# Agent attention with a gated feed-forward layer on one core: value pairs with a shared column of ones, a reciprocal column, and a new order of loads

## The reference

```python
# q, k, v: (2, 12480, 128); agents: (2, 49, 128); w_in (128, 2048), w_out (2048, 128), alpha (2048)
def sm(a, b):
    s = scale * (a @ b.transpose(0, 2, 1))
    s = s - s.max(-1, keepdims=True)
    e = np.exp(s)
    return e / (e.sum(-1, keepdims=True) + 1e-09)
agent_v = sm(agents, k) @ v
x = (sm(q, agents) @ agent_v).reshape(24960, 128)
h = x @ w_in
g = np.maximum(h, 0.0) + alpha * np.minimum(h, 0.0)
out = g @ w_out
```

## Time and profile before

| | us |
|---|---|
| median of three runs | 929.99 |
| the profiled execution | 929.73 |
| its span (first to last instruction) | 928.0 |
| PE busy | 911.3 |
| DVE busy | 627.2 |
| ACT busy | 515.1 |
| POOL busy | 108.4 |

### The profile page before, as it was taken

One profiled execution on the slowest core, in us unless ns is written; L12 is line 12 of the kernel. 1 busy time (PEld: TensorE's weight loads), 2 busy tenths in 40 slices (PEclk: granted clock), 3 DMA queues, 4 the chain that ended last, 5 costly groups with the idle time before them and its releaser, 6 DMA issues.

```text
span 928.0 us, 16051 instructions
## 1 busy us (share of the span) xinstructions
PE 911.3 (98%) x5642; PEld 488.6 (53%) x5642; DVE 627.2 (68%) x914; ACT 515.1 (56%) x695; POOL 108.4 (12%) x138
## 2 busy tenths in 40 slices
PE   8898999999999999999999999999999999999998
PEld 8874555555546556654545444444444444444443
DVE  4555666676777767767767676666767676767664
ACT  2344555556565555555556565656555555555654
POOL 5310100101001001001001010101010101010101
PEclk9998999999999999999999999999999999999999
DMA  8951222322222322211111111111111111111110
GB/s 302 301 162 50 81 77 60 101 57 67 82 71 92 99 71 89 68 36 59 35 38 54 36 59 35 58 34 54 39 52 41 49 43 45 48 40 52 41 33 22
DMA packets 74149, 65.75 MB, mean 71 GB/s; under 512 B 38528, under 2 KB 69760, under 8 KB 73856
## 3 DMA queue, kind: packets, MB, share of 16 engines
q1 hardware_dynamic: 73824, 65.19, 23.3%
q10 hardware_dynamic: 288, 0.06, 0.0%
HBM read 40.49 MB, written 12.78 MB: 57 GB/s over the span
## 4 chain that ended last, share of the span: by engine, by line
PE 93%; DMA 3%; SPq 2%; issue 2%; DVE 0%; POOLq 0%; ACT 0%
PE ps L574 55%; PE ps L557 18%; PE ps L564 7%; PE ps L538 3%; PE ps L584 2%; DMA kv_s<-kT 2%; PE ps L736 2%; PE ps L418 2%; PE ps L730 1%; PE ps L496 1%; SPq L288 1%; DMA q_s<-qT 1%; DMA PT<-stack 1%; PE ps L519 1%; PE ps L449 0%
## 5 line engine op out<-in xcount | busy, mean ns | idle before, releaser
L1142 DVE SCALAR_TENSOR_TENSOR r_lo<-ps,r_hi 128x960 f16<-128x960 f32 x416 | 466.6, 1153 | 250.8 <-ACT r_hi L897 248.4
L897 ACT ACTIVATE r_hi<-ps 128x960 f16<-128x960 f32 x416 | 386.2, 967 | 175.8 <-PE ps L564 175.7
L574 PE MATMUL ps<-r_hi,w_hi 128*128 128x480 f16 x832 | 252.4, 369 | 4.0 <-DMA q_s<-qT 3.7
L574 PE MATMUL ps<-r_hi,w_lo 128*128 128x480 f16 x832 | 248.4, 367 | 0.0
L574 PE MATMUL ps<-r_lo,w_hi 128*128 128x480 f16 x832 | 241.1, 367 | 0.0
L557 PE MATMUL ps<-PT,M_a 128*128 128x480 f16 x832 | 204.0, 367 | 0.2 <-DVE r_lo L1142 0.2
L403 POOL TENSOR_TENSOR y<-y_relu,y_lin 128x480 f32<-128x480 f32 x52 | 62.4, 1200 | 622.2 <-ACT y_relu L980 449.8
L574 PEld LDWEIGHTS ps<-r_hi,w_lo 128*128 128x128 f16 x832 | 91.4, 111 | 68.8
L557 PEld LDWEIGHTS ps<-PT,M_a 128*128 128x128 f16 x832 | 81.3, 99 | 86.8 <-DVE r_lo L1142 2.0
L574 PEld LDWEIGHTS ps<-r_lo,w_hi 128*128 128x128 f16 x832 | 85.6, 106 | 71.2
L574 PEld LDWEIGHTS ps<-r_hi,w_hi 128*128 128x128 f16 x832 | 73.0, 106 | 87.5 <-issue 43.4
(11 more groups left out here) (147 smaller groups left out, 526.1 us busy)
## 6 DMA issues: line engine op xcount, KB each, us to landing
q_s<-qT SPq DMA_DIRECT2D x52, 240.0 KB, 2.6
out<-y SPq DMA_DIRECT2D x52, 240.0 KB, 2.0
kv_s<-kT SPq DMA_DIRECT2D x24, 512.0 KB, 4.3
kv_s<-vP SPq DMA_DIRECT2D x12, 512.0 KB, 7.1
kv_s<-vS SPq DMA_DIRECT2D x8, 768.0 KB, 4.4
PR<-PT SPq DMA_DIRECT2D x156, 32.0 KB, 1.8
PT<-stack SPq DMA_TRANSPOSE x208, 2.4
w_lin<-w_out SPq DMA_DIRECT2D x1, 1024.0 KB, 8.4
```

What stands on the lines that cost most here:

```text
L574: mm = pe.matmul(ps[:, OUT, 0:CHUNK], w[:, 2 * p + u, :], r[:, s, u, :], start=(p == 0 and u == 0 and k == 0), stop=(p == PAIRS - 1 and u ...
L897: act.activation(r_hi[:, p % RING, :, :], ps[:, at:at + 2, 0:CHUNK], ACT.Relu).then_inc(hi_ready, 1)
L1142: dve.scalar_tensor_tensor(out=r_lo[:, p % RING, :, :], in0=ps[:, at:at + 2, 0:CHUNK], scalar=0.0, in1=r_hi[:, p % RING, :, :], op0=ALU.ma ...
```

## The change

Five things are changed; the diff is cut to them.

1. w_inT is loaded after the last key piece, and relu_max_row is worked after piece 11 instead of 10.
2. Tiles of values lie in pairs: a column of ones, two tiles of 128 channels, and the next pair's column of ones behind (RUN = 257). An even tile is multiplied with the ones ahead of it, an odd one with the ones behind. A load writes runs of 256 floats. The ones are written slot by slot.
3. ACT and DVE first copy the column of sums alone (den_col); PE multiplies it by `pairs` (two identity halves side by side, so that both halves' sums are added and stand on the rows of both), DVE adds EPS and takes the reciprocal of one column, scales sel by it, and turn_values multiplies by that matrix. PE's order around it and the places of the eight key tiles change.
4. SP: chunk 3 is loaded ahead of the bodies, and body n loads chunk n + 4 into its own place after q_scored(n + 3). `turn` is split: turn(0, 0), the transposes, stands ahead of k_tail and key piece (1, 0), and `spread(0, 0)`, the copies, behind them.
5. The mixes of batch 0 use other banks, the first body starts its second layer on r_low and lo_ready(1), runs second_layer(0) without key tiles, starts the second group after m_low(3), and works the key tiles in second_layer(1) and second_layer(2).

```diff
@@ -20,6 +20,7 @@
 VC = C + 1
+RUN = 2 * C + 1
 TAIL = (N - FULL * PIECE) // 2
@@ -79,9 +80,9 @@
-        kv_s = sb("kv_s", [128, 2 * RING, 8 * VC])
+        kv_s = sb("kv_s", [128, 2 * RING, 4 * RUN + 1])
         k_tail = sb("k_tail", [C, B, 2 * TAIL])
-        v_tail = sb("v_tail", [TAIL, B, 2, VC])
+        v_tail = sb("v_tail", [TAIL, B, RUN + 1])
         S = sb("S", [KT, B, TILES, A])
@@ -90,9 +91,12 @@
         rec = sb("rec", [C, A])
-        rec_sel = sb("rec_sel", [C, SEL])
-        av_rows = sb("av_rows", [128, VC])
-        den_sel = sb("den_sel", [128, SEL])
...
+        av_rows = sb("av_rows", [128, VC + 1])
+        pairs = sb("pairs", [128, 128])
+        den_col = sb("den_col", [128, 1])
+        rec_col = sb("rec_col", [128, 1])
+        rec_sel = sb("rec_sel", [128, SEL])
         av_acc = sb("av_acc", [C, A])
@@ -136,7 +140,7 @@
         W_BANK, K_BANK = 4, 5
-        F_BANK = (4, OUT, 4, 5)
+        F_BANK = (4, 4, 5, SMALL)
         REST_BANK, LIN_BANK = (OUT, SMALL), (5, SMALL)
@@ -223,12 +227,14 @@
-        def values_in(m):
-            return kv_s[:, value_slot(m), :].rearrange("p (t c) -> p t c", c=VC)
...
-        def ones_of(s):
-            return kv_s[:, s:s + RING, :].rearrange("p s (t c) -> p (s t) c", c=VC)[:, :, C:VC]
...
+        def with_ones(t):
+            at = t // 2 * RUN + t % 2 * VC
+            return slice(at, at + VC)
...
+        def without_ones(x):
+            return x.rearrange("p (j c) -> p j c", c=RUN)[:, :, 1:RUN]
@@ -248,27 +254,28 @@
                     sp.wait_ge(v_used, m - 2 * RING + 1)
-                sp.dma_start(values_in(m)[:, :, 0:C], vP[m - 1].rearrange("p (t c) -> p t c", c=C)).then_inc(in_v[(m - 1) % (2 * RING)], 16)
+                sp.dma_start(without_ones(kv_s[:, value_slot(m), 0:4 * RUN]),
+                             vP[m - 1].rearrange("p (j c) -> p j c", c=2 * C)).then_inc(in_v[(m - 1) % (2 * RING)], 16)
             def load_tail(b):
-                sp.dma_start(v_tail[:, b, :, 0:C], vTail[b].rearrange("p (t c) -> p t c", c=C)).then_inc(in_vt[b], 16)
+                sp.dma_start(v_tail[:, b, 1:RUN], vTail[b]).then_inc(in_vt[b], 16)
...
                     sp.dma_start(w_lin[:, :, :], w_out).then_inc(in_wo, 16)
-                if m == FULL - 2:
-                    sp.dma_start(w_inT_s[:, :, :], w_inT).then_inc(in_wT, 16)
+            sp.dma_start(w_inT_s[:, :, :], w_inT).then_inc(in_wT, 16)
             sp.dma_start(q_s[:, 0, :], qT[0]).then_inc(in_q[0], 16)
...
                 load_values(m)
...
-            sp.wait_ge(q_scored, 1)
-            sp.dma_start(q_s[:, 0, :], qT[2]).then_inc(in_q[0], 16)
+            for n in range(2):
...
+                sp.wait_ge(q_scored, n + 1)
+                sp.dma_start(q_s[:, n, :], qT[n + 2]).then_inc(in_q[n], 16)
@@ -287,27 +294,31 @@
+            def spread(n, half):
...
                 sp.wait_ge(q_turned, 64 * n + 64)
...
+            turn(0, 0)
...
             sp.dma_start(kv_s[:, 2, 0:PIECE], kT[1, 0]).then_inc(in_k[2], 16)
-            turn(0, 0)
+            spread(0, 0)
             for h in range(2):
...
             turn(1, 1)
+            spread(1, 1)
...
                     n = 2 * i + half
-                    if there(n + 3):
...
-                        sp.wait_ge(q_scored, n + 2)
-                        sp.dma_start(q_s[:, 1 - half, :], qT[n + 3]).then_inc(in_q[1 - half], 16)
+                    if there(n + 4):
...
+                        sp.wait_ge(q_scored, n + 3)
+                        sp.dma_start(q_s[:, half, :], qT[n + 4]).then_inc(in_q[half], 16)
                     if kind == KEYS and (not isinstance(n, int) or n + 2 + EARLY <= FULL):
@@ -324,6 +335,7 @@
                         turn(n + 2, half, n)
+                        spread(n + 2, half)
@@ -484,27 +496,29 @@
-                pe.wait_ge(ones_in, 2 if m <= RING else 3)
+                pe.wait_ge(ones_in, RING + 1 if m <= RING else 2 * RING + 1)
                 pe.wait_ge(k_exped, m + 1)
...
                     if m == 0:
-                        rhs, rows = v_tail[:, 0, t, :], TAIL
+                        rhs, rows = v_tail[:, 0, with_ones(t)], TAIL
                     else:
-                        rhs, rows = values_in(m)[:, t, :], KT
+                        rhs, rows = kv_s[:, value_slot(m), with_ones(t)], KT
...
+            def denominators_paired():
+                pe.wait_ge(b_dencol, 2)
+                pe.matmul(ps[:, K_BANK, 0:1], pairs[:, :], den_col[:, :], start=True, stop=True).then_inc(b_den, 1)
...
             def turn_values():
                 pe.wait_ge(b_rows, 2)
-                pe.matmul(ps[:, W_BANK, 0:SEL], av_rows[:, 0:C], sel[:, :], start=True, stop=True).then_inc(b_turned, 1)
...
-            def denominators_spread():
-                pe.wait_ge(b_spread, 2)
-                pe.matmul(ps[:, K_BANK, 0:SEL], ones[:, :], den_sel[:, :], start=True, stop=True).then_inc(b_den, 1)
+                pe.wait_ge(b_recsel, 1)
+                pe.matmul(ps[:, W_BANK, 0:SEL], av_rows[:, 1:VC], rec_sel[:, :], start=True, stop=True).then_inc(b_turned, 1)
@@ -590,7 +604,7 @@
                 first_scores(m)
-                if m == FULL - 2:
+                if m == FULL - 1:
@@ -636,21 +650,22 @@
+            pe.wait_ge(b_shift, 1)
+            denominators_paired()
+            pe.wait_ge(in_k[2], 16 * (FULL // RING + 1))
+            piece_scores(2, 2, range(0, 3))
...
             pe.wait_ge(wmax_ready, 1)
             turn_values()
...
-            pe.wait_ge(b_shift, 1)
-            denominators_spread()
-            pe.wait_ge(in_k[2], 16 * (FULL // RING + 1))
-            piece_scores(2, 2, range(0, 4))
+            piece_scores(2, 2, range(3, 5))
...
             value_sums(0, K_BANK)
+            piece_scores(2, 2, range(5, 8))
...
             query_scores(0)
-            piece_scores(2, 2, range(4, 8))
@@ -666,8 +681,10 @@
             mix(0, 1, F_BANK[1])
+            pe.wait_ge(l_low, 1)
             mix(0, 2, F_BANK[2])
-            pe.wait_ge(l_low, 1)
...
+            pe.wait_ge(q_shifted, 3)
             mix(0, 3, F_BANK[3])
@@ -690,7 +707,7 @@
-                        pe.wait_ge(m_low, 2)
+                        pe.wait_ge(r_low, 1)
                         pe.wait_ge(lo_ready, 1)
@@ -699,7 +716,7 @@
-                    if kind != PLAIN and not (kind == MIX_REST and half == 1):
+                    if not start and kind != PLAIN and not (kind == MIX_REST and half == 1):
                         pe.wait_ge(q_shifted, n + 3)
@@ -739,25 +756,30 @@
                         if kind == SUMS and half == 0 and t < 2:
-                            mm = pe.matmul(ps[:, SMALL, 0:A], v_tail[:, 1, t, 0:C], S[0:TAIL, 1, t, :],
+                            mm = pe.matmul(ps[:, SMALL, 0:A], v_tail[:, 1, 1 + t * C:1 + (t + 1) * C], S[0:TAIL, 1, t, :],
                                            start=(t == 0), stop=(t == 1), skip_group_check=True)
...
-                    second_layer(0, half, between)
                     if start:
+                        second_layer(0, half)
+                        pe.wait_ge(m_low, 3)
+                        second_group()
+                        pe.wait_ge(lo_ready, g + 2)
                         pe.wait_ge(m_low, 4)
-                        second_group()
-                    pe.wait_ge(lo_ready, g + 2)
-                    second_layer(1, half, lambda t: between(t + 6))
+                        second_layer(1, half, between)
+                    else:
+                        second_layer(0, half, between)
+                        pe.wait_ge(lo_ready, g + 2)
+                        second_layer(1, half, lambda t: between(t + 6))
...
                     rest_of_quad(2, half, b)
-                    second_layer(2, half)
+                    second_layer(2, half, (lambda t: between(t + 6)) if start else None)
                     pe.wait_ge(lo_ready, g + 4)
@@ -918,10 +940,8 @@
             act.wait_ge(v_used, FULL + 1)
-            act.activation(av_rows[64:64 + A, :], ps[64:64 + A, OUT, 0:VC], ACT.Copy).then_inc(b_rows, 1)
-            act.wait_ge(b_rows, 2)
-            act.activation(den_sel[64:64 + A, :], sel[64:64 + A, :], ACT.Copy,
-                           scale=av_rows[64:64 + A, C:VC]).then_inc(b_spread, 1)
+            act.activation(den_col[64:64 + A, :], ps[64:64 + A, OUT, C:VC], ACT.Copy).then_inc(b_dencol, 1)
+            act.activation(av_rows[64:64 + A, 1:VC + 1], ps[64:64 + A, OUT, 0:VC], ACT.Copy).then_inc(b_rows, 1)
             query_hi(1)
@@ -1146,17 +1166,20 @@
             then(dve.memset(sel[:, :], 0.0))
-            then(dve.memset(den_sel[:, :], 0.0))
+            then(dve.memset(den_col[:, :], 0.0))
...
-            dve.memset(ones_of(RING), 1.0).then_inc(ones_in, 1)
-            dve.memset(v_tail[:, 0, :, C:VC], 1.0).then_inc(ones_in, 1)
+            for s in range(RING, 2 * RING):
+                dve.memset(kv_s[:, s, 0:4 * RUN + 1:RUN], 1.0).then_inc(ones_in, 1)
```

(22 more changed lines are left out.)

## The result

Twenty runs of each kernel gave 930.29 us before (median, 927.43 to 936.95) and 927.36 us after (925.58 to 929.41). The ratio is 0.9963, with a 95% interval of 0.9948 to 0.9978. The change makes the kernel faster, by 0.4%: the forecast of 921.1 and its range (918.8 to 924.8) were too low.

What follows compares the result with a forecast made beforehand. PE bounds the kernel, busy 98% of the span, so only time ahead of 90 us can be won: 2.6 (parts 1 to 3) + 6.3 (part 5) = 8.9 us off 929.73, 920.8, against the median 921.1; range 918.8 to 924.8.

Steps and rivals of the forecast that it cites:

- the forecast case: Whole kernel: 8.9 us won, 921.1 us, with the clock staying up behind the new waits; chance 0.5.
- rival 1: Near 53 to 56 us: the clock falls at the new waits, price 1.85 us, time 923.0; chance 0.18.
- what is late next: SP's order: Transposes ahead of k_tail and key piece (1, 0): PE waits 1.0 and 1.1 us; parts 1 to 3 bring 2.6, not 4.5.
- part 5: First body, queries four ahead: the 3.5 us wait and the slow stretch behind it go, 6.3 us won (3.5 to 6.8).
- part 1: Key stage, w_inT last among the keys: turn_weights starts at 29.6 instead of 33.3, 3.7 us early.
- Part 2: Value loads in 1024 B runs: near 330 GB/s, 1.6 us a piece instead of 1.8, and SP's queue freed.
- Rival 2: Value loads stay at 290 GB/s and SP stays blocked: parts 1 to 3 bring 0.2 us, time 923.5; chance 0.15.
- Part 3: Tail scores to first mix, reciprocal as a column: 4.4 us instead of 5.2, 0.8 won if nothing else is late.
- Part 4: First mixes and layers, reordered banks and key tiles: gives 0.1 us and mostly fills gaps.
- rival 4: Every later body: SP's new wait delays turn(n+2); at 0.4 us per chunk the kernel takes 941; chance 0.02.

Runs made afterwards that it cites:

- the fillers: The changed kernel with 13 float32 matmuls that nobody reads ahead of the waits for k_tail and key piece (1, 0): 922.99 us, ratio 0.9907 to the kernel before.
- the loads ahead: The changed kernel with k_tail and key piece (1, 0) issued ahead of turn(0, 0): 920.39 us, ratio 0.9896 to before; run once more, 924.52 us.
- the repeat: The changed kernel run once more, nothing altered: 927.16 us, ratio 0.9962 to the kernel before.
- the earlier slot: The kernel with the loads ahead, key piece (1, 0) waiting for v_used 8 instead of 9: 920.51 us, ratio 0.9879 to before; run once more, 920.64 us.
- queries alone: The kernel before with only the queries loaded four chunks ahead: 923.26 us, ratio 0.9928 to the kernel before.
- w_inT back: The kernel with the loads ahead, w_inT back behind key piece 10 and relu_max_row behind piece 10: 921.91 us, ratio 0.9885 to the kernel before.

## Why the prediction was wrong

**The failed step: the forecast case had the clock stay up behind the two new waits.** That it falls was rival 1. The forecast had the two waits, their place and their cause right (what is late next: SP's order), and then asked whether the clock would fall behind them, gave that 0.18 and 1.85 us, and took the other case. It fell in 31 of the change's 32 timed runs, by their mean granted clock, and cost about 4.2 us: 927.2 against 923.0 with the fillers, and 11.9 against 7.6 us from the key piece to the second mix (with the loads ahead). The price of 1.85 was read off pieces 11 and 12, where the low stretch of the earlier trace rows had lasted three microseconds; here it lasts ten. A better guide stood in the forecast's own part 5, from the earlier trace rows: behind the wait of 3.51 us PE took 6.6 us for what takes it 3.35 one chunk later, a price of 3.25. And the evidence against, that 1.43 us of waiting had left the clock alone, was two thirds of the idling now forecast; 2.1 us in two parts was nearer the 2.57 that had been followed by a fall.

**The second miss is the sizes in SP's order**, which decide how long PE idles. k_tail's issue took 1.31 us behind the transposes for 0.43, and with the shorter shift of the block the key piece came at 59.18 for 55.85: 3.3 us. About 1.8 of them are part 1's. SP was through with its value and query loads at 48.33 and began the transposes at 48.51, 1.1 us later than that shift explains (45.6 + 1.8); the transposes then took 0.5 us less than forecast, and k_tail's issue 0.9 more. At the second mix these 3.3 us and the 4.3 of the clock make up the 7.4 between the forecast and the measurement to within 0.2.

**Part 1** (w_inT last) was taken at 3.7 us. turn_weights starts 1.9 us early in the profile after and 2.3 in the repeat. In the kernels with no other delay PE still waits 0.2 to 1.5 us for w_inT and starts at 30.2 to 32.0, so it lands 0.8 to 2.6 us later than the 29.4 worked out. The sum counted all of the earlier trace rows's 5.44 us, of which 1.6 were the clock (3.81 where it did not fall); without that fall w_inT's place moves turn_weights by no more than the profiles scatter, 0.6 us for 30.90. The experiment that puts it back shows no measurable loss.

**Part 2** was right: 359, 347 and 350 GB/s in three stretches for 330 forecast, and without the longer runs the kernel with the loads ahead falls back to the change's own time. Whether the runs also free SP's queue, as the forecast took it, the profiles don't tell: the stretch of the two q loads holds a wait for the second scores, too. Rival 2, the rule of the Trainium skill ("DMA: Bandwidth & Descriptors", Specifications) that 512 bytes are enough, is not borne out here: from 33 to 42 us the loads moved 275 to 293 GB/s with runs of 512 bytes (kernel before and the experiment), 347 to 359 with 1024 (kernel after).

**Part 3** was hidden, as forecast: the column's scaling is ready 1.2 us before the key piece. With the loads ahead the first mix starts at 59.83, 3.7 us behind the key piece; the sum had 59.85 and 3.95. That the two starts meet is chance: this kernel has another order on SP and starts its block 1.3 us later than forecast (30.90 for 29.6). In the second profile of the kernel with the earlier slot, where PE waits only 0.20 us for the key piece, the stretch from the tail scores to the first mix takes 4.1 us, for 5.2 before and 4.4 in the sum. No kernel leaves out part 3 alone, so its worth in the time is not shown.

**Part 4** was taken at 0.1 us. From the first rest of a quad to second_layer(4) it is 15.45 us with the old order (queries alone, 66.10 to 81.55) and 15.42 with the new one (70.77 to 86.19): nothing.

**Part 5** was right: taken at 6.3 us, it shows as 6.0 in the stretch and as 7.2 in the medians of queries alone, interval 4.7 to 8.7. The new wait on SP cost nothing, and rival 4 is out.

In sum: at the second mix the change, forecast 2.6 us early, is 4.8 us late (71.08 for 66.24). From there to second_layer(4) it wins 6.0. That leaves 1.2 us there and 1.7 in the spans of the two profiles, 2.9 in the medians, of 8.9 forecast.

What stays open: what decides whether the clock falls behind a wait of 1.1 to 2.6 us. It did in some runs and not in others of one program.

## What to carry to other kernels

When several loads and transposes share one issuing queue, price the queue: a transpose held it for 1.3 us here, and four of them ahead of a load that PE waits for cost more than the start won. A wait of PE has a second price, the clock behind it, and it can be the larger; where the profile shows one fall behind a similar wait, forecast it. Where a wait can't be taken out, matmuls that nobody reads are a cheap test of which price is being paid, and here a cure.

## What the runs showed of the hardware

- The low level of the clock, once entered, lasted 3.4 us (29.3 to 32.7, kernel before), 6.8 us (80.5 to 87.3, the same), ten us (59 to 69, kernel after), again 6.8 (27.8 to 34.6, w_inT back) and 3.4 (60.5 to 63.9, queries alone), though PE was busy nearly all through.
- Behind waits of 3.0 to 4.1 us in sum it fell in every profile, and by the mean clock in 31 of 32 runs of the change; behind one of 2.2 to 2.6 us ahead of key piece 11 it fell in two of three profiles, behind 1.1 to 1.4 us near 58 us in two of four (not behind 1.43 in the kernel before, but behind 1.05 in queries alone). Behind the waits of 0.2 to 1.5 us for w_inT near 31 us it fell in none of ten. So the length of a wait alone does not tell. The runs of one program can then form two groups, 4 us apart, and the mean granted clock of a run (0.996 against 0.999) tells to which it belongs.
- Value loads with 1024-byte runs moved 1.2 times the bytes per second of those with 512-byte runs (359 against 291 GB/s in 33 to 36 us).
- The key piece took 3.5 to 4.4 us from issue to landing in the five profiles in which it is issued behind the first transposes. Ahead of them it took 5.4 to 6.8 us in seven, 4.7 in the kernel before and 3.2 with w_inT back. Whether the transposes or the query loads around it lengthen it is open.
- The issue of k_tail held SP's queue for 1.31, 1.57 and 1.65 us behind the transposes, but for 0.58 there in the kernel with fillers, and for 1.22 ahead of them in one profile with the loads ahead (0.43 in its repeat).
